# Computing h transposed in the expert stage of a fused fp32 kernel on one Trainium2 core

## The reference, cut to what matters

```python
N, D, E, F = (4608, 512, 8, 1024)
for e in range(E):
    mask = expert_idx == e
    h = np.maximum(x[mask] @ w1[e], 0.0)          # [tokens, 512] @ [512, 1024]
    out[mask] = gate_w[mask, None] * (h @ w2[e])  # [tokens, 1024] @ [1024, 512]
```

## Time and profile before

| | |
|---|---|
| median of 3 runs | 1454.56 us |
| profiled execution | 1453.83 us, span 1452.1 us |
| mean granted TensorE clock | 0.972 of full speed |
| PE busy, PEld busy | 1365.4 us (94%), 1119.7 us (77%) |
| DVE, ACT, POOL busy | 662.7 us (46%), 398.8 us (27%), 190.0 us (13%) |
| DMA | 112.58 MB, mean 78 GB/s |

### The profile page before, as it was taken

How to read it: one execution, slowest core, us unless ns; L and a number is a source line. 1 busy time by engine, 2 the same in 40 slices (tenths; PEclk the granted TensorE clock), 3 DMA queues, 4 the chain that set the end, 5 groups by cost and what they waited for, 6 DMA issues and landing times.

```text
span 1452.1 us, 18961 instructions
## 1 busy us (share of the span) xinstructions
PE 1365.4 (94%) x6730; PEld 1119.7 (77%) x6731; DVE 662.7 (46%) x947; ACT 398.8 (27%) x632; POOL 190.0 (13%) x234
## 2 busy tenths in 40 slices
PE   4998489999979999994999999999999999999998
PEld 3877378888868888883887878878788787887887
DVE  4677543222545435255545444353444535444343
ACT  5887122111333313234212121121211212112121
POOL 4564112111212222121000000000000000000000
PEclk8999689999989999997999999999999999999999
DMA  7785243111435324144101000010100101001000
GB/s 281 262 262 175 65 156 119 43 43 44 152 111 192 101 101 159 43 155 133 52 1 58 0 29 29 0 58 0 47 11 0 58 0 56 2 0 58 0 30 15
DMA packets 71484, 112.58 MB, mean 78 GB/s; under 512 B 6817, under 2 KB 38561, under 8 KB 70817
## 3 DMA queue, kind: packets, MB, share of 16 engines
q1 hardware_dynamic: 64192, 91.79, 18.7%
q0 software_dynamic: 6112, 19.93, 4.0%
q10 hardware_dynamic: 1152, 0.52, 0.2%
HBM read 84.17 MB, written 27.53 MB: 77 GB/s over the span
## 4 chain that ended last, share of the span: by engine, by line
PE 86%; DVE 5%; ACT 3%; DMA 2%; issue 2%; SPq 2%; POOL 0%; ACTq 0%; DVEq 0%; POOLq 0%
PE ps L320 9%; PE ps L322 9%; PE ps L321 9%; PE ps_o L322 7%; PE ps_o L320 7%; PE ps_o L321 7%; PE ps_h L320 5%; PE ps_h L322 5%; PE ps_h L321 5%; PE ps_y L320 5%; PE ps_y L322 5%; PE ps_y L321 5%; PE ps_hT L1240 2%; SPq L431 2%; PE ps_sr L1132 1%
## 5 line engine op out<-in xcount | busy, mean ns | idle before, releaser
L320 PE MATMUL ps<-yT_hi,w_hi 128*128 128x512 f32 (+1 forms) x576 | 221.8, 385 | 23.1 <-DVE yT_lo L1034 23.1
L758 ACT ACTIVATE gT_hi<-act_g 128x512 fp32r<-128x512 f32 (+1 forms) x144 | 87.7, 609 | 563.6 <-DVE act_g L1047 563.6
L1044 DVE TENSOR_SCALAR neg<-ps,alpha 128x512 f32<-128x512 f32 (+1 forms) x144 | 103.7, 720 | 292.9 <-PE ps L322 292.9
L322 PE MATMUL ps<-yT_hi,w_lo 128*128 128x512 f32 (+1 forms) x576 | 221.0, 384 | 0.0
L321 PE MATMUL ps<-yT_lo,w_hi 128*128 128x512 f32 (+1 forms) x576 | 220.8, 383 | 0.0
L322 PE MATMUL ps_o<-w_hi,gT_lo 128*128 128x512 f32 x544 | 212.3, 390 | 0.0
L320 PE MATMUL ps_o<-w_hi,gT_hi 128*128 128x512 f32 x544 | 211.9, 389 | 0.0
L321 PE MATMUL ps_o<-w_lo,gT_hi 128*128 128x512 f32 x544 | 211.8, 389 | 0.0
L320 PEld LDWEIGHTS ps<-yT_hi,w_hi 128*128 128x128 f32 x576 | 108.6, 189 | 49.2 <-DVE yT_lo L1034 26.2
L1050 DVE TENSOR_TENSOR gT_lo<-act_g,gT_hi 128x512 fp32r<-128x512 f32 (+1 forms) x144 | 95.4, 663 | 97.2 <-ACT gT_hi L758 97.2
L320 PE MATMUL ps_h<-w_hi,xgT_hi 128*128 128x512 f32 x296 | 122.3, 413 | 11.7 <-DVE w_lo L789 7.7
(11 more groups left out here) (189 smaller groups left out, 1741.2 us busy)
## 6 DMA issues: line engine op xcount, KB each, us to landing
stage<-in_moe_w SPq DMA_DIRECT2D x32, 1024.0 KB
xs_all<-in_xT SPq DMA_DIRECT2D x8, 1024.0 KB, 6.4
xN_all<-in_xN SPq DMA_DIRECT2D x8, 1024.0 KB, 6.0
rows_x<-xrow SPq DMA_DIRECT2D x32, 256.0 KB, 2.5
yg<-rows_y SPq DMA_DIRECT2D x128, 64.0 KB, 1.9
out_rows<-orow SPq DMA_DIRECT2D x32, 256.0 KB, 2.1
stage<-in_moe_w_in SPq DMA_DIRECT2D x4, 1024.0 KB
stage<-in_moe_w_out SPq DMA_DIRECT2D x4, 1024.0 KB
```

The source lines that it names most:

```text
L320: pe.matmul(out, s_hi, m_hi, start=start, stop=False)
L322: return pe.matmul(out, s_lo, m_hi, start=False, stop=stop)
L758: act.activation(gT_hi[:, c % 2, f, 0:w], act_g[:, 0:w], ACT.Copy).then_inc(g_hi_ready, 1)
L1044: dve.tensor_scalar(neg[:, 0:w], ps_1[f][:, 0:w], 0.0, alpha[:, ft:ft + 1], ALU.min, ALU.mult)\
```

## The change

h is computed transposed from the start. The stationary operand is now a 128x128 block of the first matrix, and the 128 tokens of the slot move. Each half of h is 4 blocks of hidden units (j) x 4 blocks of model columns (k) x 3 matmuls, and each of these moves 128 columns instead of 512. So a slot has 96 matmuls for h where it had 24. What stands in `ps_h[c]` is what stood in `ps_hT[c]`. VectorE's copy, TensorE's eight transposes of h, two PSUM tiles and two semaphores go. Relu and rest read `ps_h` directly. TensorE's order is: half 0, half 1, the transposes of the next x, all of `result`.

```diff
             def slot(s):
                 for c in range(2):
-                    act.wait_ge(hT_ready, 2 * s + c + 1)
-                    act.activation(hidT_hi[:, c, :, :], ps_hT[c][:], ACT.Relu).then_inc(hT_hi_ready, 1)
+                    act.wait_ge(h_ready, 2 * s + c + 1)
+                    act.activation(hidT_hi[:, c, :, :], ps_h[c][:], ACT.Relu).then_inc(hT_hi_ready, 1)
...
                 for c in range(2):
-                    dve.wait_ge(h_ready, 2 * s + c + 1)
-                    dve.tensor_copy(hid[:, c, :], ps_h[c][:]).then_inc(h_copied, 1)
                     dve.wait_ge(hT_hi_ready, 2 * s + c + 1)
-                    dve.scalar_tensor_tensor(out=hidT_lo[:, c, :, :], in0=ps_hT[c][:], scalar=0.0,
+                    dve.scalar_tensor_tensor(out=hidT_lo[:, c, :, :], in0=ps_h[c][:], scalar=0.0,
...
-            def transpose_h(s, c):
-                pe.wait_ge(h_copied, 2 * s + c + 1)
-                for k in range(KF // 2):
-                    mm = pe.transpose(ps_hT[c][:, k, :], hid[:, c, k * P:(k + 1) * P], ident[:])
-                mm.then_inc(hT_ready, 1)
-
-            def hidden(c, ks, buf):
-                for k in ks:
-                    mm = three(pe, ps_h[c][:], xgT_hi[:, k, :], xgT_lo[:, k, :],
-                               w_first(w_hi[buf], k, c * F // 2, F // 2), w_first(w_lo[buf], k, c * F // 2, F // 2),
-                               k == 0, k == KD - 1)
+            def hidden(c, buf):
+                for j in range(KF // 2):
+                    f = c * KF // 2 + j
+                    for k in range(KD):
+                        mm = three(pe, ps_h[c][:, j, :], w_first(w_hi[buf], k, f * P, P), w_first(w_lo[buf], k, f * P, P),
+                                   xgT_hi[:, k, :], xgT_lo[:, k, :], k == 0, k == KD - 1)
                 return mm
...
             def slot(s, buf):
                 pe.wait_ge(xT_lo_ready, s + 1)
-                hidden(0, range(KD), buf).then_inc(h_ready, 1)
-                hidden(1, range(0, 2), buf)
-                transpose_h(s, 0)
-                hidden(1, range(2, KD), buf).then_inc(h_ready, 1)
+                hidden(0, buf).then_inc(h_ready, 1)
+                hidden(1, buf).then_inc(h_ready, 1)
                 transpose_x(s + 1)
                 pe.wait_ge(yrow_ready, s + 1)
-                pe.wait_ge(hT_lo_ready, 2 * s + 1)
-                result(0, range(0, 1), buf)
-                transpose_h(s, 1)
-                result(0, range(1, KF // 2), buf)
-                pe.wait_ge(hT_lo_ready, 2 * s + 2)
-                result(1, range(KF // 2), buf).then_inc(y_ready, 1)
+                for c in range(2):
+                    pe.wait_ge(hT_lo_ready, 2 * s + c + 1)
+                    y = result(c, range(KF // 2), buf)
+                y.then_inc(y_ready, 1)
```

More of the change, by code:

```diff
@@ L203, in build @@
         xgT_lo = sb("xgT_lo", [P, KD, P], F32R, c=sc)
-        hid = sb("hid", [P, 2, F // 2], c=sc)
         hidT_hi = sb("hidT_hi", [P, 2, KF // 2, P], F32R, c=sc)
@@ L233, in build @@
         pc = ExitStack()
-        ps_h = [pb(f"ps_h{i}", [P, F // 2], c=pc) for i in range(2)]
-        ps_hT = [pb(f"ps_hT{i}", [P, KF // 2, P], c=pc) for i in range(2)]
+        ps_h = [pb(f"ps_h{i}", [P, KF // 2, P], c=pc) for i in range(2)]
         ps_xT = pb("ps_xT", [P, KD, P], c=pc)
@@ L277, in build @@
         xT_hi_ready, xT_lo_ready = sem("xT_hi_ready"), sem("xT_lo_ready")
-        h_ready, h_copied, hT_ready = sem("h_ready"), sem("h_copied"), sem("hT_ready")
+        h_ready = sem("h_ready")
         hT_hi_ready, hT_lo_ready = sem("hT_hi_ready"), sem("hT_lo_ready")
@@ L1225, in _ @@
             for _ in range(14):
-                pe.matmul(ps_h[1][:], w_hi[0][:, 0:P], w_hi[0][:, 0:DM], start=True, stop=True)
+                pe.matmul(ps_h[1][:].rearrange("p k t -> p (k t)"), w_hi[0][:, 0:P], w_hi[0][:, 0:DM], start=True, stop=True)
             pe.wait_ge(index_ready, 5)
@@ L1280, in _ @@
                         slot(s, par)
-                    pe.matmul(ps_h[0][:, 0:P], ident[:], ident[:], start=True, stop=True).then_inc(expert_done, 1)
+                    pe.matmul(ps_h[0][:, 0, :], ident[:], ident[:], start=True, stop=True).then_inc(expert_done, 1)
             def up(g, c, w):
```

## The result

The changed kernel takes 1631.47 us (median of 4 runs, 1630.17 to 1631.81) against 1454.49 us for the kernel before on the same chip: a ratio of 1.1216, 95% interval 1.1197 to 1.1236. It is 177.0 us slower. The forecast was 1607 us, with a range of 1572 to 1650: the sign holds, the time lies in the range, and the load sets the pair as the prediction said. But 19 us of the 177 came from a step that it had priced at nothing (a low clock in two slots), and 5 from the size of a load and its matmul (0.1113 us for 0.110).

What follows compares the result with a forecast made beforehand. TensorE, busy 94% of the span, was taken as the bound. Per slot 10.56 - 5.55 - 0.88 = +4.13 us, times 37 = +152.8 on 1453.83 gives 1606.6, with the median 0.7 higher 1607 us; range 1572 to 1650.

Steps and rivals of the forecast that it cites:

- What goes: Per slot on TensorE: 24 512-column matmuls for h, 5.55 us, and two groups of transposes, 0.88 us; VectorE's copies count nothing.
- What comes: Per slot on TensorE: 96 128-column matmuls for h, each bound by its load at 0.110 us, 10.56 us in all.
- Waits that come or go: Handovers to result and next x are covered, 7.7 us weights gap stays, low clock after standstills costs the same: nothing added.
- a step of h outside 0.103 to 0.118: Sign of being wrong: the matmul-and-load pairs of h stepping outside these bounds, in us.
- Granted clock 1.00 in the same stretches: Expected in the changed profile: TensorE at full clock in the expert-stage stretches that had it before.
- the 0.118 bound of the load: Upper bound for a pair in h, from 256-column matmuls: 11.33 us for h, 28 us more in all, 1636.
- small things a slot: Changes of kind and queue supply at 37 slots, 0.1 to 0.2 us a slot, widening 1582 to 1636 to 1572 to 1650.
- The clock falls: Rival: chip grants 1.2 GHz through h, pairs step by 0.214, +14.1 us a slot, +522, 1977 us; chance 5%.
- Loads fully hidden: Rival: in h only columns bind, 0.061 us a pair, -0.57 us a slot, -21 us, 1433 us, faster; chance 5%.
- partly hidden: Rival: pairs of h step halfway between columns and load, 0.082 us, +1.44 us a slot, 1508 us; chance 3%.
- A lower rate of narrow fp32r matmuls: Rival: in h 128 columns cost what 512 do, 0.231 us a pair, +15.7 us a slot, +581, 2036 us; chance 6%.

Runs made afterwards that it cites:

- e1: Kernel before without the eight transposes of h and VectorE's copies, relu and rest reading ps_h untransposed: 1420.64 us, ratio 0.9764.
- e2: Changed kernel with 256 instead of 128 moving columns in each of the 96 matmuls of h, same loads: 1637.82 us, ratio 1.1256.
- e3: Changed kernel with 64 instead of 128 moving columns in each of the 96 matmuls of h, same loads: 1900.15 us, ratio 1.3059.
- e4: Changed kernel without the third product of h, 64 matmuls a slot for h instead of 96: 1494.28 us, ratio 1.027.
- e8: Changed kernel with discarded 512-column matmuls (2 + 18, and 34) in the expert stage's two standstills, under half a microsecond of pause left: 1606.07 us.
- e5: Changed kernel with discarded 512-column matmuls (2 + 12, and 28) in the expert stage's two standstills, pauses of 1.5 and 1.3 us left: 1621.89 us.
- e6: Kernel before with discarded 512-column matmuls in the expert stage's two standstills (2 + 12, and 28) and 46 ahead of the dense stage: 1449.16 us.
- e9: Kernel before with 18, 34 and 54 discarded wide matmuls in three standstills, plus 36 ahead of the 34 index matmuls: 1449.62 us.

## Why the prediction came out as it did

**What goes** held: 0.88 us a slot for two groups of transposes, 0.86 by e1.

**What comes** held in its mechanism: the load sets the pair (the step of the changed kernel itself, e2, e3, e4). The size was 0.110 for a measured 0.1113. That is 0.12 us a slot and 4.6 us in all; with it the sum of warm slots is 157.4 against 157.9 read from the periods.

**Waits that come or go** failed in one sentence: that at the first slot and after the gap the clock "is low for a few us", "which costs the same before and after". I had the two steps right (0.214 a pair from L1085) but took the length of the low stretch over from the kernel before, as if it ran from the standstill by time alone. It ends when wide matmuls have run for a while: 4.8 us of them in the kernel before, 4.0 in the changed one. In the changed kernel none come until h is through. The first slot, from its first h matmul to `yrow`, takes 28.9 us for 14.9, and the period across the wait for weights 36.58 for 22.94. That is 14.0 and 13.6 us more, where a warm slot of the same kind has 4.2 and 4.3 more: 9.8 + 9.3 = 19.1 us that the forecast had at nothing. 157.9 + 19.1 = 177.0, the difference measured. By the prediction's own sign of being wrong, a step of h outside 0.103 to 0.118, these two slots with 0.213 are a miss, and "Granted clock 1.00 in the same stretches" failed in the first of them.

**What was luck.** The time lies in the range, 1572 to 1650, but no term of the range was about the clock. Its upper part came from the 0.118 bound of the load and from small things a slot, and the missing 19 us happened to fit in there. e8, without the low clock in these slots, lands on 1606 us against the 1607 forecast. That too is partly chance: the pair was sized 4.6 us too low in all, and e8 saves about as much that the kernel before pays for the low clock in its own two slots, and that the forecast had kept.

**The rivals.** *The clock falls* was the nearest to the miss. I set it at 5% and as an affair of all slots or none. It looked in the right direction: with equal loads, e2 and e3 changed the columns, and the clock came out otherwise. But the evidence against it was 3.15 us at full clock. That shows that a clock is held for so long and says nothing on whether it is regained; and e3 was at full clock for 5.5 us of narrow work before it fell. *Loads fully hidden* and *partly hidden* are refuted by the measured step, 0.1113 where they wanted 0.061 and 0.082, and the sharing of a load by e4. *A lower rate of narrow fp32r matmuls* wanted 0.231 and is refuted by the same step, and by e3's 0.11 at 64 columns. Of the two statements of the Trainium skill ("TensorE: Matmul & The Clock Gate"), the one that a load takes its columns over 1.2 GHz ("LDWEIGHTS (loading the stationary operand)") gives 107 ns here and the trace 111 at full clock, 213 at half; the 81 ns at N=128 ("Back-to-back issue gap") is in no run.

## What to carry to other kernels

In these runs an fp32r matmul with its 128x128 load steps by 0.111 us at 64 and 128 moving columns, 0.118 at 256 and 0.231 at 512. From these I estimate that the load binds up to about 250 columns: swapping operands to save a transpose pays only if the moving side stays wide. Here two groups of four transposes at 0.44 us a group were saved, and h went from 24 x 0.231 = 5.5 us a slot to 96 x 0.111 = 10.7.

And price a stretch at low clock by what TensorE does after the pause, not by the pause: the 96 narrow pairs kept the low clock for all their length. Discarded wide matmuls put into a standstill cost nothing here and took the low clock away (25 us in the changed kernel, 5.9 in the kernel before). Ahead of narrow work they had to reach right up to it; ahead of wide work a pause of 1.4 us did no harm in the profiled execution, and one of 2.2 us lost the clock.

## What the runs showed of the hardware that I had not expected

After a standstill, 96 pairs of 128 columns ran 20 us at 1.2 GHz without regaining 2.4, while 256 columns with the same loads regained it 4.5 us into h. With 64 columns the clock fell from 2.4 to 1.2 GHz in the middle of unbroken work with PEld at 100%. Pauses of 1.5 and 1.3 us ahead of 128-column work lost it in both places in the profiled execution of e5, and by the times in one of them in two other executions; pauses as long ahead of 512-column work (e6) did not. And 34 bf16 matmuls of 86 columns took 5.4 us with the clock at 1.2 GHz throughout and with it at 2.4 for the first 3 us (e9).
